# Attention and two experts in one kernel: a transposition moved by one step, a subtraction doubled, a store put ahead of a load

## The chip, the cores and the metric

One core of a Trainium2 chip runs the whole kernel. The metric is device microseconds of one execution. Engines are TensorE (PE, with PEld for its weight loads), VectorE (DVE), ScalarE (ACT), GpSimd (POOL) and SyncE (SP), which here only issues DMAs.

## What is computed

A recurrent attention over 768 time steps, for 4 x 8 heads of dimension 40, and behind it two dense experts over the 3072 tokens:

```python
for t in range(S):
    y[:, :, t] = einsum('bhd,bhde->bhe', rt, state)
    Sa = einsum('bhde,bhe->bhd', state, at)
    state = state * wt - einsum('bhd,bhe->bhde', Sa, bt) + einsum('bhd,bhe->bhde', vt, kt)
x = y as (3072, 320)
x = ((x @ w1) * (x @ w2)) @ w3 @ w_out          # 320 -> 1024 -> 1024 -> 320
out = relu(x @ w_in) ** 2 @ w_out2              # 320 -> 2048 -> 320
```

## The kernel before

**Attention** runs in 24 windows of 64 time steps; a window covers two of the four batches, 16 heads as 8 pairs. In a window the recurrence becomes triangular systems. VectorE scales and masks the operands (`scale_a`, `scale_bk`, `mask_ak`), `fill_lanes` spreads the 32x32 diagonal blocks over lanes, GpSimd inverts them there step by step (`invert`, 62 small instructions), and `turn_inverse(n)` on VectorE transposes the inverse of window n back into `invT`. TensorE multiplies by it in `make_u0(n)` and `make_u1(n)`. On TensorE `make_u0(n)` waits for `turn_inverse(n)` and also for `mask_ak(n+1)`.

**The experts** run in 6 tiles of 512 tokens. The first expert folds `w3 @ w_out` into one matrix, so that it has 8 hidden blocks (`a0` to `a7`, `b0` to `b7`) and its fold; the second has 16 hidden blocks (`c0` to `c15`) and its projection. Every value is split in a high and a low part (`_hi`, `_lo`) rounded to the fp32r format, and a product is summed from the parts. For a hidden block ScalarE takes a copy (`take`, into `left`), VectorE combines (`combine`), ScalarE rounds (`h_hi`), VectorE subtracts (`rest_hidden`, `h_lo`), and TensorE uses it two blocks later. `into_hidden` sums eight terms, the last with `x_lo` of the third block. The model dimension is 320, 2 x 128 + 64. Of the third block `x2T_hi` holds its 64 rows twice, in partitions 0 to 63 and 64 to 127; of the weights the lower half of these partitions holds the high part and the upper half the low part. `x2T_lo` holds the 64 low rows in partitions 0 to 63 and zeros above them.

**The order of work** is written out by hand. Each engine has a generator `experts()`, which yields 56 times in a tile, and a loop over windows 4 to 23 that draws 14 steps of it in each window with `next(beside)`. The first LEAD = 4 steps are empty. Windows 0 to 3 (the opening) stand before the loop, with the folding of `w3 @ w_out`. So the middle of a tile, where the first expert's result is turned into `x2T_hi` and `x2T_lo`, falls at the end of windows 5, 9, 13, 17 and 21, directly ahead of the next window's `scale_a`; the sixth tile's middle comes behind the windows.

**Weights** are rounded and split in the first tile, and written to DRAM for later tiles. A list `splits` gives each split a slot. SP issues all DMAs in its own order; `load_staged` brings raw weights into one of four `stage` buffers, four splits ahead (LOOK); ScalarE (`round_split`) and VectorE (`rest_of_split`) split them into `w_ring` or `v_ring`; `store_split` writes the result to `gate_rows`, `win_rows` or `wout_rows`. `pass_split(x)` on SP does both: the next load into the stage that x used, and the store of x. A load for a `w` split is four DMAs, for a `v` split one.

Lines that the text names: L1486 the transposition of `turn_inverse`; L1452 `scale_a` (`azk`); L1459 `scale_bk` (`bkT`); L1467 and L1471 `mask_ak`; L1556 and L1558 `combine`; L1250 and L1548 `h_hi` and `h_lo`; L1564 `rest_x`; L1590 the low part of the third block; L1239 `round_split` of a `v` split; L1535 and L1540 to L1542 `rest_of_split`; L866 `into_hidden`; L768 `make_u0` and `make_u1`; L811 `turn_uv`; L388 and L394 to L397 `load_staged`; L410 to L419 `store_split`; L429 `load_w`.

Of the kernel before, what the change touches and what calls it, by code (L numbers as in the profile page):

```python
# [5 lines left out]
F32 = mybir.dt.float32  # L6
F32R = mybir.dt.float32r
ALU = mybir.AluOpType
# [69 lines left out]
def attention_with_experts(nc, xT_dram, inputs, w1, w2, w3, w_out, w_in, w_out2, out):  # L78


    P, C, X, DP = 128, inputs.C, inputs.PAIRS, 64
# [7 lines left out]
    TOK = 512  # L89
    SUB, TILES = TOK // P, T // TOK  # L90
    REM = M - 2 * P
    DX = M + REM
    FT, FT2 = F // P, F2 // P
# [7 lines left out]
    OPENING = 4  # L101
# [12 lines left out]
    with ExitStack() as ctx:  # L114
# [3 lines left out]
        def sem(name):  # L118
            return ctx.enter_context(nc.semaphore(name))
# [84 lines left out]
        w_loaded = [sem(f"w_loaded{x}") for x in range(SLOTS)]  # L204
        v_loaded = [sem(f"v_loaded{x}") for x in range(SLOTS)]
        x_loaded, x_rounded, x_split = sem("x_loaded"), sem("x_rounded"), sem("x_split")
        third_rounded, third_split, third_cleared = sem("third_rounded"), sem("third_split"), sem("third_cleared")
        taken, combined, hi_made, lo_made, h_used, out_stored = (
            sem("taken"), sem("combined"), sem("hi_made"), sem("lo_made"), sem("h_used"), sem("out_stored"))

# [136 lines left out]
        def _(sp):  # L347
# [104 lines left out]
            W_LOADS, V_LOADS = TILES * (FT + FT2 // 2), TILES * (FT + FT2)  # L452

            def pass_split(x):
                _, kind, at = splits[x]
                if x + LOOK < len(splits):
                    sp.wait_ge(v_split if kind else w_split, at - FT + 1 if kind else at + 1)
                    load_staged(FT + x + LOOK)
                store_split(x)

            def split_first():
                for t, _ in enumerate(experts()):
# [223 lines left out]
        def _(pe):  # L686
# [273 lines left out]
            def experts():  # L960
                for _ in range(LEAD):
                    yield
                pe.wait_ge(y_scaled, OPENING)
                pe.wait_ge(st_copied, OPENING)
                for i in range(TILES):
                    def wait_x2(n):
                        if n in (0, 2):
                            wait_first_reader(pe, f"x{n // 2}", i)
                        elif n in (4, 5):
                            wait_drained(pe, f"x{n - 4}", i)  # L970
                        elif n == 6:
                            pe.wait_ge(third_rounded, 2 * (i + 1))
                        elif n == 7:
                            pe.wait_ge(third_split, i + 1)
                            pe.wait_ge(third_cleared, 1)

                    def wait_x(n):
                        if n in (0, 2):
                            pe.wait_ge(x_rounded, 3 * i + n // 2 + 1)
                        elif n in (4, 5):  # L980
                            pe.wait_ge(x_split, 3 * i + n - 3)
                        elif n == 6:
                            pe.wait_ge(x_rounded, 3 * (i + 1))
                        elif n == 7:
                            pe.wait_ge(x_split, 3 * (i + 1))

                    for f in range(FT + LAG):
                        if f < FT:
                            at = (FT + FT2 // 2) * i + f
                            wait_w(at)  # L990
                            for n, use in enumerate((f"a{f}", f"b{f}")):
                                (wait_left, wait_right)[n](f, i)
                                into_hidden(use, w_ring[at % SLOTS], 5 * P * n, xT_hi, xT_lo,
                                            *((wait_x,) if use == "a0" else ()))
                                yield
                        if f >= LAG:
                            fold(f - LAG, i)
                            yield
                    for f in range(FT2 + LAG):
                        if f < FT2:  # L1000
                            at = (FT + FT2 // 2) * i + FT + f // 2
                            wait_w(at)
                            wait_hidden(f, i)
                            into_hidden(f"c{f}", w_ring[at % SLOTS], 5 * P * (f % 2), x2T_hi, x2T_lo,
                                        *((wait_x2,) if f == 0 else ()))
                            yield
                        if f >= LAG:
                            project(f - LAG, i)
                            yield
# [152 lines left out]
        def _(act):  # L1162
# [158 lines left out]
                last = nc.scalar.copy(unit_rows[rows], ident[rows, rows].rearrange("i (x r) -> i x r", r=4).unsqueeze(  # L1321
                    3).broadcast_to([BLK, X, 4, X]))
            last.then_inc(unit_placed, 1)

            act.wait_ge(padded, 6)
            nc.scalar.copy(x2T_lo[REM:P, 2, :], zeros[REM:P].broadcast_to([REM, TOK])).then_inc(third_cleared, 1)
            copy_r(0)
            copy_w3(0)
            copy_blocks(0)
# [96 lines left out]
        def _(dve):  # L1426
# [140 lines left out]
            def experts():  # L1567
                for _ in range(LEAD):
                    yield
                for i in range(TILES):  # L1570
                    for f in range(FT + LAG):
                        if f < FT:
                            if 0 < f <= LAG:
                                rest_hidden(f - 1, i)
                            yield
                            combine(f, i)
                            yield
                        if f >= LAG:
                            if f < FT:
                                rest_hidden(f, i)  # L1580
                            if f == FT + LAG - 1:
                                wait_first_reader(dve, "x2", i)
                                drain(nc.vector.tensor_tensor(third[:], bank("x2")[0:REM], third[:], ALU.add), "x2", 1)
                                for m in range(2):
                                    wait_first_reader(dve, f"x{m}", i)
                                    drain(nc.vector.tensor_tensor(x2T_lo[:, m, :], bank(f"x{m}"),  # L1586
                                                                  x2T_hi[:, m, :].bitcast(F32), ALU.subtract),
                                          f"x{m}", 1)
                                dve.wait_ge(third_rounded, 2 * i + 1)
                                nc.vector.tensor_tensor(x2T_lo[0:REM, 2, :], third[:], x2T_hi[0:REM, 2, :].bitcast(F32),  # L1590
                                                        ALU.subtract).then_inc(third_split, 1)
                            yield
                    for f in range(FT2 + LAG):
                        if f < FT2:
                            if 0 < f <= LAG:
                                rest_hidden(FT + f - 1, i)
                            combine(FT + f, i)
                            yield
                        if f >= LAG:
                            if f < FT2:  # L1600
                                rest_hidden(FT + f, i)
                            if f == FT2 and i + 1 < TILES:
                                rest_x(i + 1)
                            if f == FT2 + LAG - 1:
                                wait(dve, out_stored, 16 * i)
                                for s in (1, 3):
                                    wait_filled(dve, f"o{s}", i)
                                    drain(nc.vector.tensor_copy(out_rows[:, s, :], bank(f"o{s}")[:, 0:M]), f"o{s}")
                            yield
# [84 lines left out]
            scale_a(5)  # L1694
            rest_of_fold(7)
            scale_bk(5)
            turn_inverse(OPENING)
            rest_x(0)
            for n in range(OPENING, WINDOWS):
                one, two = window_steps(n)  # L1700
                if OPENING < n and one:
                    scale_a(n + 1)
                next(beside)
                next(beside)
                if OPENING < n and one:
                    scale_bk(n + 1)
                next(beside)
                if one:
                    mask_ak(n + 1)
                    fill_lanes(n + 1)  # L1710
                next(beside)
                next(beside)
                next(beside)
                next(beside)
                add_x1(n)
                if two:
                    scan(n + 2)
                next(beside)
                if two:
                    invert_decay(n + 2, 0)  # L1720
                next(beside)
                if two:
                    invert_decay(n + 2, 1)
                next(beside)
                if two:
                    new_state(n)
                next(beside)
                mask_read(n)
                next(beside)
                scale_y(n)  # L1730
                next(beside)
                if one:
                    turn_inverse(n + 1)
                next(beside)
            for _ in beside:
                pass
# [31 lines left out]
```

## Time and profile before

| | before |
|---|---|
| median of 3 runs | 1060.74 us (1056.57 to 1061.88) |
| profiled execution | 1060.74 us, span 1059.0 us |
| TensorE busy | 1023.2 us, 97% |
| VectorE busy | 634.7 us, 60% |
| ScalarE busy | 419.7 us, 40% |
| GpSimd busy | 486.1 us, 46% |
| TensorE's granted clock, mean | 0.99 of full |

The profile is of one execution. A timeline row gives the start and the duration in us, the engine, the line, the operation with its output and inputs, and, in brackets, how long the engine had been idle before and what ended that. Where a row says x2 or x3, that many instructions are merged into it. A stretch's row gives its length, the busy time (and instructions) of PE, PEld, DVE, ACT and POOL, the granted clock, the busy share of the DMA engines and the GB/s that they moved.

### The profile page before, as it was taken

How to read it: one execution, taken by the hardware profiler on the slowest of the kernel's cores; microseconds unless marked ns; L12 is line 12 of the kernel's file. 1: busy time of each engine (PE TensorE's matmuls, PEld its weight loads, DVE VectorE, ACT ScalarE, POOL GpSimd, SP SyncE). 2: the span in 40 equal slices, each digit the busy share in tenths (PEclk: the TensorE clock that was granted, in tenths of full speed). 3: DMA queues.
4: the chain of work that ended last, by engine and by line, in shares of the span. 5: the costliest groups of instructions: out<-in, count | busy, mean ns of one | idle time of the engine just before them, and what ended most of it. 6: DMA issues, size and time to landing. Idle time of an engine off the chain costs nothing.

```text
span 1059.0 us, 27606 instructions
## 1 busy us (share of the span) xinstructions
PE 1023.2 (97%) x11008; PEld 880.8 (83%) x11008; DVE 634.7 (60%) x1005; ACT 419.7 (40%) x796; POOL 486.1 (46%) x1573
## 2 busy tenths in 40 slices
PE   5998989999999999999999999999999999999998
PEld 5786768779898888898888898888988888897797
DVE  6876366777875656666567566467567555442333
ACT  3453434454543343443344343334434234332332
POOL 4777755527447346346346355355365364200000
PEclk8997999999999999999999999999999999999999
DMA  9953556756886764757665757756648744555552
GB/s 177 188 127 65 155 132 170 197 165 203 226 234 178 170 150 126 180 145 180 151 157 131 176 140 202 150 134 155 160 125 217 154 117 132 154 169 184 166 170 75
DMA packets 267390, 169.05 MB, mean 160 GB/s; under 512 B 199680, under 2 KB 229376, under 8 KB 267264
## 3 DMA queue, kind: packets, MB, share of 16 engines
q1 hardware_dynamic: 267264, 167.29, 62.7%
q8 instruction: 88, 1.44, 0.6%
q14 instruction: 38, 0.31, 0.1%
HBM read 141.03 MB, written 26.21 MB: 158 GB/s over the span
## 4 chain that ended last, share of the span: by engine, by line
PE 79%; DVE 4%; ACT 2%; issue 1%; ACTq 0%; DVEq 0%
PE aside L866 31%; PE moe_bank L953 16%; PE moe_bank L938 8%; PE both L830 3%; PE both L730 3%; PE both L768 3%; PE both L840 2%; PE both L844 2%; PE both L760 2%; PE both L811 2%; PE both L743 1%; PE both L819 1%; PE both L793 1%; PE both L853 1%; PE both L716 1%
## 5 line engine op out<-in xcount | busy, mean ns | idle before, releaser
L671 POOL TENSOR_TENSOR inv_tmp<-blk,inv 128x60 f32<-128x60 f32 (+24 forms) x744 | 209.5, 282 | 358.4 <-DVE blk L1480 301.4
L675 POOL TENSOR_TENSOR inv<-inv,inv_tmp 128x60 f32<-128x60 f32 (+24 forms) x744 | 237.4, 319 | 58.3
L953 PE MATMUL moe_bank<-v_ring,h_hi 128*128 128x320 f32 x768 | 175.3, 315 | 0.0
L866 PE MATMUL aside<-x2T_hi,w_ring 128*128 128x512 f32 x480 | 148.0, 405 | 4.4 <-DVE h_lo L1548 4.3
L866 PE MATMUL aside<-xT_hi,w_ring 128*128 128x512 f32 x480 | 148.2, 406 | 2.2 <-DVE h_lo L1548 1.5
L1558 DVE SCALAR_TENSOR_TENSOR aside<-aside,left 128x512 f32<-128x512 f32 x96 | 66.9, 697 | 122.0 <-ACT left L1258 122.0
L953 PEld LDWEIGHTS moe_bank<-v_ring,h_hi 128*128 128x128 f32 x768 | 128.0, 188 | 3.9
L1548 DVE TENSOR_TENSOR h_lo<-aside,h_hi 128x512 fp32r<-128x512 f32 x144 | 97.4, 677 | 49.7 <-ACT h_hi L1250 49.0
L1250 ACT CAST h_hi<-aside 128x512 fp32r<-128x512 f32 x144 | 84.7, 588 | 94.9 <-DVE aside L1558 49.6
L953 PE MATMUL moe_bank<-v_ring,h_lo 128*128 128x320 f32 x384 | 118.6, 309 | 0.0
L1258 ACT ACTIVATE left<-aside 128x512 f32<-128x512 f32 x96 | 57.4, 598 | 117.3 <-PE aside L866 117.3
L866 PEld LDWEIGHTS aside<-x2T_hi,w_ring 128*128 128x128 f32 x480 | 84.1, 188 | 21.3 <-issue 6.3
L866 PEld LDWEIGHTS aside<-xT_hi,w_ring 128*128 128x128 f32 x480 | 84.7, 188 | 19.2 <-DVE h_lo L1548 2.6
L866 PE MATMUL aside<-xT_lo,w_ring 128*128 128x512 f32 x288 | 97.1, 391 | 0.0
L866 PE MATMUL aside<-x2T_lo,w_ring 128*128 128x512 f32 x288 | 96.9, 391 | 0.0
L1438 DVE RECIPROCAL undecay<-decay 104x256 f32<-104x256 f32 x48 | 83.2, 1739 | 0.2
L938 PE MATMUL moe_bank<-h_hi,v_ring 128*128 128x512 f32 x240 | 81.4, 404 | 0.0
L953 PEld LDWEIGHTS moe_bank<-v_ring,h_lo 128*128 128x128 f32 x384 | 72.1, 188 | 0.0
L1556 DVE TENSOR_TENSOR aside<-left,aside 128x512 f32<-128x512 f32 x48 | 33.0, 687 | 63.1 <-PE aside L866 63.1
L866 PEld LDWEIGHTS aside<-xT_lo,w_ring 128*128 128x128 f32 x288 | 54.1, 188 | 12.8 <-DVE xT_lo L1564 0.6
L866 PEld LDWEIGHTS aside<-x2T_lo,w_ring 128*128 128x128 f32 x288 | 54.1, 188 | 12.3 <-DVE x2T_lo L1586 0.2
L1197 ACT COPY uv<-both 32x320 f32<-32x320 f32 x88 | 36.8, 418 | 68.9 <-PE both L768 63.4
(151 smaller groups left out, 1604.2 us busy)
## 6 DMA issues: line engine op xcount, KB each, us to landing
w_ring<-gate_rows SPq DMA_DIRECT2D x40, 640.0 KB, 4.6
w_ring<-win_rows SPq DMA_DIRECT2D x40, 640.0 KB, 4.1
v_ring<-wout_rows SPq DMA_DIRECT2D x80, 320.0 KB, 3.1
v_ring<-fold_rows SPq DMA_DIRECT2D x48, 320.0 KB, 4.2
gate_rows<-w_ring SPq DMA_DIRECT2D x8, 640.0 KB, 6.4
win_rows<-w_ring SPq DMA_DIRECT2D x8, 640.0 KB, 4.4
wout_rows<-v_ring SPq DMA_DIRECT2D x16, 320.0 KB, 5.9
stage<-in_moe_w SPq DMA_DIRECT2D x8, 512.0 KB
```

The costliest lines, as they stand in the source:

```text
L671: nc.gpsimd.tensor_tensor(tmp, x[:, j, 0:j].unsqueeze(2).broadcast_to([P, j, X - lo]), mine[:, j:j + 1, lo:X].broadcast_to([P, j, X - lo]) ...
L675: nc.gpsimd.tensor_tensor(mine[:, 0:j, lo:X], mine[:, 0:j, lo:X], tmp, ALU.add).then_inc(solve, 1)
L866: last = nc.tensor.matmul(bank(use), w, x, start=n == 0, stop=n == len(terms) - 1)
L938: last = nc.tensor.matmul(bank(f"x{m}"), weights[:, lo:lo + P], h[at % RING][:], start=f == 0 and n == 0, stop=f == FT - 1 and n == len(te ...
L953: last = nc.tensor.matmul(bank(f"o{s}")[:, 0:M], h[at % RING][:, s * P:(s + 1) * P], weights[:, rest * M:(rest + 1) * M], start=f == 0 and ...
L1197: last = nc.scalar.copy(uv[n % 2][rows, :, q, 0:D], by_head(its_first(n), rows))
L1250: nc.scalar.copy(h_hi[at % RING][:], hidden_at(x)).then_inc(hi_made, 1)
L1258: nc.scalar.activation(left[x % 2][:], hidden_at(x), ACT.Relu).then_inc(taken, 1)
L1438: nc.vector.reciprocal(undecay[0:E, xs], decay[n % 4][0:E, xs, 1:C + 1]).then_inc(undecayed, 1)
L1548: nc.vector.tensor_tensor(h_lo[at % RING][:], hidden_at(x), h_hi[at % RING][:].bitcast(F32), ALU.subtract).then_inc(lo_made, 1)
L1556: nc.vector.tensor_tensor(into, left[x % 2][:], into, ALU.mult).then_inc(combined, 1)
L1558: nc.vector.scalar_tensor_tensor(out=into, in0=into, scalar=0.0, in1=left[x % 2][:], op0=ALU.max, op1=ALU.mult).then_inc(combined, 1)
```

## The change

Four edits.

- `x2T_lo` of the third block is no longer zero in partitions 64 to 127. VectorE writes the 64 low rows a second time, there; ScalarE's copy of zeros at the start, with its semaphore `third_cleared`, is gone, and `third_split` counts two for each tile. TensorE's last term then adds the product of both low parts as well.
- In `pass_split` the store of split x is issued before the staged load of x + 4.
- `turn_inverse(n)` in the window loop moves from the end of window n-1 (between its last two steps) to window n, behind `scale_a(n+1)` and one step.
- `turn_inverse(4)`, which stood ahead of `rest_x(0)`, is now the first of these, in window 4, behind `rest_x(0)`.

```diff
--- before.py
+++ after.py
@@ -204,7 +204,7 @@
         w_loaded = [sem(f"w_loaded{x}") for x in range(SLOTS)]
         v_loaded = [sem(f"v_loaded{x}") for x in range(SLOTS)]
         x_loaded, x_rounded, x_split = sem("x_loaded"), sem("x_rounded"), sem("x_split")
-        third_rounded, third_split, third_cleared = sem("third_rounded"), sem("third_split"), sem("third_cleared")
+        third_rounded, third_split = sem("third_rounded"), sem("third_split")
         taken, combined, hi_made, lo_made, h_used, out_stored = (
             sem("taken"), sem("combined"), sem("hi_made"), sem("lo_made"), sem("h_used"), sem("out_stored"))
 
@@ -452,11 +452,9 @@
             W_LOADS, V_LOADS = TILES * (FT + FT2 // 2), TILES * (FT + FT2)
 
             def pass_split(x):
-                _, kind, at = splits[x]
+                store_split(x)
                 if x + LOOK < len(splits):
-                    sp.wait_ge(v_split if kind else w_split, at - FT + 1 if kind else at + 1)
                     load_staged(FT + x + LOOK)
-                store_split(x)
 
             def split_first():
                 for t, _ in enumerate(experts()):
@@ -971,8 +969,7 @@
                         elif n == 6:
                             pe.wait_ge(third_rounded, 2 * (i + 1))
                         elif n == 7:
-                            pe.wait_ge(third_split, i + 1)
-                            pe.wait_ge(third_cleared, 1)
+                            pe.wait_ge(third_split, 2 * (i + 1))
 
                     def wait_x(n):
                         if n in (0, 2):
@@ -1321,9 +1318,6 @@
                 last = nc.scalar.copy(unit_rows[rows], ident[rows, rows].rearrange("i (x r) -> i x r", r=4).unsqueeze(
                     3).broadcast_to([BLK, X, 4, X]))
             last.then_inc(unit_placed, 1)
-
-            act.wait_ge(padded, 6)
-            nc.scalar.copy(x2T_lo[REM:P, 2, :], zeros[REM:P].broadcast_to([REM, TOK])).then_inc(third_cleared, 1)
             copy_r(0)
             copy_w3(0)
             copy_blocks(0)
@@ -1587,8 +1581,10 @@
                                                                   x2T_hi[:, m, :].bitcast(F32), ALU.subtract),
                                           f"x{m}", 1)
                                 dve.wait_ge(third_rounded, 2 * i + 1)
-                                nc.vector.tensor_tensor(x2T_lo[0:REM, 2, :], third[:], x2T_hi[0:REM, 2, :].bitcast(F32),
-                                                        ALU.subtract).then_inc(third_split, 1)
+                                for q in range(2):
+                                    nc.vector.tensor_tensor(x2T_lo[REM * q:REM * (q + 1), 2, :], third[:],
+                                                            x2T_hi[0:REM, 2, :].bitcast(F32), ALU.subtract).then_inc(
+                                                                third_split, 1)
                             yield
                     for f in range(FT2 + LAG):
                         if f < FT2:
@@ -1694,13 +1690,13 @@
             scale_a(5)
             rest_of_fold(7)
             scale_bk(5)
-            turn_inverse(OPENING)
             rest_x(0)
             for n in range(OPENING, WINDOWS):
                 one, two = window_steps(n)
                 if OPENING < n and one:
                     scale_a(n + 1)
                 next(beside)
+                turn_inverse(n)
                 next(beside)
                 if OPENING < n and one:
                     scale_bk(n + 1)
@@ -1729,8 +1725,6 @@
                 next(beside)
                 scale_y(n)
                 next(beside)
-                if one:
-                    turn_inverse(n + 1)
                 next(beside)
             for _ in beside:
                 pass
```

## Rows read from the trace of the kernel before

**Rows 1.** The page, part 4: shares of the span in the chain that ended last.
```profile
PE 79%; DVE 4%; ACT 2%; issue 1%; ACTq 0%; DVEq 0%
```

**Rows 2.** The transpositions by tile (ns min/median/max), and the waits: us, times, longest.
```profile
L1486 DVE STREAM_TRANSPOSE invT<-inv x24: 656/688/715, 46.2 to 910.1; 128x256 f32<-128x256 f32 x24
...
DVE invT L1486 <- POOL inv L675: 6.1, 2, 4.7
...
PE both L730 <- DVE bkT L1459: 3.9, 4, 1.3
```

**Rows 3.** VectorE's timeline at two window edges: start, duration, instruction, [idle before].
```profile
426.20 0.70 DVE L1558 SCALAR_TENSOR_TENSOR aside<-aside,left 128x512 f32<-128x512 f32 x1 [2.58 <-ACT left L1258]
426.81 0.68 DVE L1486 STREAM_TRANSPOSE invT<-inv 128x256 f32<-128x256 f32 x1
427.56 0.69 DVE L1548 TENSOR_TENSOR h_lo<-aside,h_hi 128x512 fp32r<-128x512 f32 x1
...
350.61 0.70 DVE L1556 TENSOR_TENSOR aside<-left,aside 128x512 f32<-128x512 f32 x1 [2.32 <-PE aside L866]
```

**Rows 4.** Timelines of VectorE and TensorE in the middle of the second tile.
```profile
387.82 0.68 DVE L1590 TENSOR_TENSOR x2T_lo<-third,x2T_hi 64x512 fp32r<-64x512 f32 x1
388.43 1.40 DVE L1452 SCALAR_TENSOR_TENSOR azk<-both,decay 64x512 f32<-64x512 f32 x2
390.24 0.70 DVE L1558 SCALAR_TENSOR_TENSOR aside<-aside,left 128x512 f32<-128x512 f32 x1 [0.41 <-ACT left L1258]
391.60 0.69 DVE L1548 TENSOR_TENSOR h_lo<-aside,h_hi 128x512 fp32r<-128x512 f32 x1 [0.66 <-ACT h_hi L1250]
...
388.85 0.40 PE L866 MATMUL aside<-x2T_lo,w_ring 128*128 128x512 f32 x1
...
392.43 1.17 PE L866 MATMUL aside<-x2T_hi,w_ring 128*128 128x512 f32 x4 [0.49 <-DVE h_lo L1548]
```

**Rows 5.** Timelines of VectorE and TensorE where the opening ends.
```profile
145.60 1.90 DVE L1564 TENSOR_TENSOR xT_lo<-x_raw,xT_hi 128x512 fp32r<-128x512 f32 x3 [2.15 <-ACT xT_hi L1265]
147.53 0.86 DVE L1467 COPY diag<-both 32x256 f32<-32x256 f32 x2
...
150.07 0.76 PE L768 MATMUL both<-x_row,invT 32*32 32x40 f32 x32 [2.01 <-DVE azk L1471]
```

**Rows 6.** VectorE's timeline around a weight split in the first tile.
```profile
156.84 0.69 DVE L1540 TENSOR_TENSOR w_ring<-stage,w_ring 128x512 fp32r<-128x512 f32 x1 [1.31 <-ACT w_ring L1242]
157.55 0.45 DVE L1542 TENSOR_TENSOR w_ring<-stage,w_ring 64x256 fp32r<-64x256 f32 x1
158.03 0.99 DVE L1493 TENSOR_TENSOR x_row<-both,x_row 32x320 f32<-32x320 f32 x2
```

**Rows 7.** Timelines in the middle of the first tile and of the last.
```profile
222.96 0.49 DVE L1535 TENSOR_TENSOR v_ring<-stage,v_ring 128x320 fp32r<-128x320 f32 x1 [0.36 <-ACT v_ring L1239]
...
996.50 0.67 DVE L1590 TENSOR_TENSOR x2T_lo<-third,x2T_hi 64x512 fp32r<-64x512 f32 x1
...
997.40 0.39 PE L866 MATMUL aside<-x2T_lo,w_ring 128*128 128x512 f32 x1
```

**Rows 8.** Timelines of SP's queue, ScalarE and TensorE, a wait, and the stretch 286 to 289.
```profile
282.57 0.43 SPq L388 DMA_DIRECT2D stage<-in_moe_w_out  x1
283.05 0.43 SPq L419 DMA_DIRECT2D win_rows<-w_ring  x1
...
287.57 0.46 ACT L1239 CAST v_ring<-stage 128x320 fp32r<-128x320 f32 x1 [2.30 <-DMA stage<-in_moe_w_out]
288.05 0.85 ACT L1197 COPY uv<-both 32x320 f32<-32x320 f32 x2
...
289.00 1.05 PE L811 MATMUL both<-ident,uv 128*104 128x128 f32 x8 [0.51 <-issue]
...
ACT v_ring L1239 <- DMA stage<-in_moe_w_out: 2.3, 1, 2.3
...
286.00:289.00 3.00, 2.49 (x36) 1.81 (x29) 2.96 (x8) 1.37 (x4) 2.53 (x7) 1.00 1.01 373
```

## The prediction

> **What bounds the kernel now.** I read the page first, then the waits, then the timelines of the engines around each place that the diff touches. The page's chain that ended last is TensorE's for 79% of the span, VectorE's for 4% and ScalarE's for 2% [rows 1]. So a VectorE or ScalarE instruction matters only where TensorE stands still behind it; the question for each edit is whether it lands in a gap of VectorE or ahead of something TensorE waits for. In the timeline of TensorE, idle times over 0.2 us are few after 145 us, and they recur. One comes at every middle of a token tile, when the second expert's `c2` waits for `h_lo` of `c0` (0.49 us in four tiles, [rows 4]); the others are in the opening and in the first tile, where the weights are also split.
>
> The profiled execution took 1060.74 us, 1059.0 of them span; it is also the median of the three runs (1056.57 to 1061.88), so I add to 1060.74.
>
> **The change part by part.**
>
> *The transposition `turn_inverse`, moved in the window loop.* It takes about 0.69 us, 24 times [rows 2]. Before, it stood ahead of the last beside-step of window n-1; now it stands behind `scale_a(n+1)` and one beside-step of window n. Old place: in the windows that end inside the second expert it sits between `combine` and `rest_hidden`, where VectorE has to wait for ScalarE's rounding. In [rows 3], `combine` starts at 426.20, the transposition at 426.81, `h_lo` at 427.56: 1.36 us from combine to `h_lo`. At 390.24 there is no transposition and `h_lo` starts at 391.60, again 1.36 us [rows 4]. So it costs nothing where it is. New place: for window starts that fall in the second expert the first beside-step of the window is again a `combine`, and the next begins with `rest_hidden`, so the same gap takes it. For the window starts inside the first expert the step behind it is a `combine` that VectorE waits 2.32 us for [rows 3]. Cost nothing, gain nothing; without that cover it would be 0.6 us for each of 19 windows, 11 us. Its reader, `make_u0(n)`, waits for `mask_ak(n+1)` anyway, and that stands behind the transposition on VectorE in both orders, so no new wait comes in. VectorE's waits for GpSimd's inversion are 6.1 us in total, two of them [rows 2]; the longer one (4.7 us) is in the opening before the loop and stays, the other comes at the end of a first-expert stage, ahead of the wait for ScalarE's copy of `third`, so removing it frees nobody.
>
> *The same transposition in the opening.* `turn_inverse(4)` stood ahead of `rest_x(0)`. There VectorE idled 2.15 us for ScalarE's `xT_hi` [rows 5], so it was free. Now it comes behind `rest_x(0)` and in front of `mask_ak(5)`, with only empty steps between (LEAD is 4). `mask_ak(5)` starts at 147.53 directly behind the last `xT_lo`, and TensorE's `make_u0(4)` at 150.07 has been idle 2.01 us for exactly that result (`azk`, L1471) [rows 5]. One transposition, started back to back, is 0.6 us: **+0.6 us**, all exposed.
>
> *A second subtraction for the last 64 rows of `x2T_lo`, six times.* It replaces one ScalarE copy of zeros at the start, when TensorE still waits for its first DMA: gain nothing. The existing subtraction takes 0.68 us (387.82 in [rows 4]), and the instruction after it starts 0.61 us later, since the two overlap. The new one writes partitions 64 to 127. [Rows 6] shows a pair of that kind: an op of 0.69 us, the one on partitions 64 to 127 starting 0.71 us later, and the next 0.48 us after that for a duration of 0.45: no overlap into it, none out of it. So I count 0.80 us until the next VectorE instruction, not 0.61. (The Trainium skill, VectorE: DVE Perf Modes, section "Two Vector instructions with no wait between them", gives a model in which an instruction whose output begins in another quadrant of partitions than the last one's is held until the earlier ones have finished; [rows 6] agrees. If it did not hold here, the four middle tiles would cost 0.6 us each in place of 0.8.)
> What waits behind it, in the four middle tiles: TensorE's eighth term of `c0`, which started at 388.85 with the old subtraction finished at 388.50, must wait until about 389.25 (0.4 us); and `scale_a`, which moves from 388.43 to 389.23. ScalarE's second `copy_r` piece needs the first half of `scale_a`, and `take(c0)` is queued behind it on ScalarE, then `combine` (390.24), `h_hi`, `h_lo` (391.60), then TensorE's `c2` at 392.43, which already waits 0.49 us [rows 4]. That whole chain moves by 0.8, so **4 x 0.8 = +3.2 us**. In the first tile a weight split lies between, for which VectorE idled 0.36 us [rows 7]: 0.70 less 0.36, **+0.35 us**. In the last tile there is no `scale_a`: the subtraction at 996.50 ends at 997.17, the second would end at about 997.86, and TensorE's term started at 997.40 [rows 7]: **+0.5 us**.
>
> *The order in `pass_split`: store before next load.* The same waits, and the same issues on SP's queue: a store moves ahead of one or four loads. Every store comes 0.5 to 2 us earlier; in the trace nobody waits for one of these stores. Every staged load is issued one store later and its bytes line up behind the store's. ScalarE rounds staged weights 32 times and idles for a load before one of them alone [rows 8]: that load was issued at 282.57 and rounded at 287.57 after 2.30 us of idling for it. The copies of `uv` for which `turn_uv` waits are queued behind that rounding (288.05), and TensorE starts `turn_uv` at 289.00 after 0.51 us idle. So this delay is exposed already. With the new order the 640 KB store of `win_rows` (now issued at 283.05) goes in front of the load: 655,360 B at the 373 GB/s that the row of this stretch shows are 1.8 us, with the DMA engines as good as full (1.01) [rows 8]. I take **+1.8 us**; bounds are 0 (bytes of both interleave and the load still lands in time) and 4 (this load and the next one both late by as much). (The Trainium skill, DMA: Bandwidth & Descriptors, section "Queues, rings and completion order", says that each DMA engine takes the descriptors of a ring in order, which would put the load fully behind the store; the wait at 287.57 fits that but doesn't prove it.)
>
> **Sum:** 0.6 + 3.2 + 0.35 + 0.5 + 1.8 = 6.45 us. 1060.74 + 6.45 = **1067.2 us**, 0.6% slower. A measurement of this kernel can tell about 0.5% (5.3 us) from no change, so this lies just beyond the line.
>
> **Rivals.**
> 1. *The load isn't held up by the store.* For it: the two directions differ, and the load before took no more than 5 us in all. Against: saturated engines. Then 4.65 us remain: 1065.4, within 0.5%.
> 2. *The added subtraction is half covered.* TensorE waits only for its own eighth term (0.4 us at 388.85) and ScalarE's chain catches up, because the second `copy_r` piece has slack. Against it: `azk` starts without a gap at 388.43. Then 4 x 0.4 in place of 4 x 0.8: 1065.6; with rival 1 together 1063.8. Within 0.5%.
> 3. *More staged loads come late.* In the first tile the waits of SP's queue leave some loads little time, as this one shows, and only the latest is seen in the waits of before; if three of them become late by a store each (1.8 us), the time is 1067.2 + 3.6 = 1070.8.
> 4. *Faster, by taking the transposition out of the end of the window.* If it delays `scale_a` and with it `bkT` and `cross`, TensorE's waits for `bkT` go, 3.9 us in four places [rows 2]; with all 6.1 us of VectorE's waits for GpSimd given back as well that is 10.0 us, less the 4.65 above: 1055.4. It decides if the transposition that waited for GpSimd inside the loop holds up `scale_a` and the chain to `c2`. Against it: VectorE idles for ScalarE or TensorE in the gaps where the transpositions stand [rows 3].
>
> **How the numbers follow.** Forecast (load late, subtraction exposed) 0.44, of which 0.38 over the line of 5.3 us; rival 1 0.19; rival 2, alone or with 1, 0.18; rival 3 0.11; rival 4 0.08. Slower by over 0.5%: 0.38 + 0.11 = 0.49. Within 0.5%: 0.06 + 0.19 + 0.18 = 0.43. Faster by over 0.5%: 0.08, rival 4, whose full price just reaches the line. The range leaves out rival 4 and the top of rival 3: 1061.5 (rivals 1 and 2 together, less half the spread of the runs before) to 1071.0. The forecast's own range is 1065.5 to 1069.
>
> **What would show it.** In the profile after: TensorE's wait before `c2` in the middle tiles grows from 0.49 to about 0.9 us, plus about 0.4 us before the eighth term of `c0`, both behind VectorE; `azk` starts about 1.4 us behind the first of the two subtractions instead of 0.6. The wait before `make_u0(4)` goes from 2.01 to 2.6 us. `h_lo` still starts 1.36 us behind `combine` where the transposition now lies between. ScalarE's wait for the staged output weights goes from 2.3 to about 4 us and TensorE's wait before that `turn_uv` from 0.5 to 2.3. The prediction is wrong if the middle-tile wait stays near 0.5, if the staged wait stays or goes, or if a transposition shows up in front of something TensorE waits for.

## The result and the profile after

The changed kernel takes 1068.25 us (median of 6 runs, 1066.61 to 1071.19) against 1060.6 us before (6 runs, 1056.57 to 1061.88): ratio 1.0081, 95% interval 1.0057 to 1.0105. In a second series it gave 1069.42 us against 1061.49, ratio 1.0088 (1.0068 to 1.0109). It is slower, by 8.6 to 9.3 us by the ratios (7.7 and 7.9 by the medians) where 6.45 were forecast. The profiled execution after took 1071.43 us, 1069.6 of them span, so it is above all six of its own runs, and differences read from it are at their upper end.

The page of the changed kernel, its engines and the chain that ended last:

```profile
PE 1026.7 (96%) x11008; PEld 882.2 (82%) x11008; DVE 639.1 (60%) x1011; ACT 418.8 (39%) x795; POOL 483.7 (45%) x1573
...
PE 78%; DVE 5%; issue 2%; ACT 1%; ACTq 0%; DVEq 0%
```

TensorE has the same instructions and stands still for longer; VectorE has six more, ScalarE one less. In the chain TensorE and ScalarE have one point less each, VectorE and "issue" (time in which an engine waits for nothing that the profile shows) one more ([rows 1] for before).

The largest single loss in this profile does not come from VectorE. Timelines of SP's queue, of ScalarE and of TensorE in the changed kernel, where [rows 8] are those of before, and the two stretches that follow:

```profile
282.69 0.58 SPq L429 DMA_DIRECT2D w_ring<-gate_rows  x1
283.32 0.43 SPq L419 DMA_DIRECT2D win_rows<-w_ring  x1
283.79 0.47 SPq L388 DMA_DIRECT2D stage<-in_moe_w_out  x1
...
291.79 0.46 ACT L1236 CAST v_ring<-stage 128x320 fp32r<-128x320 f32 x1 [6.51 <-DMA stage<-in_moe_w_out]
292.27 0.85 ACT L1194 COPY uv<-both 32x320 f32<-32x320 f32 x2
...
293.22 1.92 PE L809 MATMUL both<-ident,uv 128*104 128x128 f32 x8 [4.72 <-issue]
...
292.00:299.00 7.00, 5.78 (x46) 5.43 (x48) 5.48 (x6) 3.54 (x7) 5.67 (x18) 0.51 0.85 309
299.00:1060.00 761.00, 754.62 (x7801) 653.88 (x7796) 434.11 (x669) 288.37 (x543) 298.52 (x991) 1.00 0.60 156
```

The store is issued ahead of the load now. The load, issued at 283.79, is rounded by ScalarE 8.0 us later, 5.0 before; ScalarE idles 6.51 us for it instead of 2.30, and TensorE stands still for 4.72 us instead of 0.51. Then comes something that was not in the forecast: TensorE's granted clock, at full speed before (2.4 GHz), is 0.51 in the stretch from 292 to 299, so about 1.2 GHz, and full again from 299 on. The eight transpositions at 293.22 take 1.92 us; those of before at 289.00 took 1.05 [rows 8].

The middle of the second tile, timelines of VectorE and TensorE in the changed kernel ([rows 4] for before):

```profile
394.53 1.40 DVE L1585 TENSOR_TENSOR x2T_lo<-third,x2T_hi 64x512 fp32r<-64x512 f32 x2
395.97 1.41 DVE L1446 SCALAR_TENSOR_TENSOR azk<-both,decay 64x512 f32<-64x512 f32 x2
397.79 0.70 DVE L1552 SCALAR_TENSOR_TENSOR aside<-aside,left 128x512 f32<-128x512 f32 x1 [0.41 <-ACT left L1255]
398.52 0.67 DVE L1480 STREAM_TRANSPOSE invT<-inv 128x256 f32<-128x256 f32 x1
399.15 0.69 DVE L1542 TENSOR_TENSOR h_lo<-aside,h_hi 128x512 fp32r<-128x512 f32 x1
...
395.99 0.50 PE L864 MATMUL aside<-x2T_lo,w_ring 128*128 128x512 f32 x1 [0.26 <-DVE x2T_lo L1585]
399.99 1.17 PE L864 MATMUL aside<-x2T_hi,w_ring 128*128 128x512 f32 x4 [0.79 <-DVE h_lo L1542]
```

From the first subtraction to `azk` it is 1.44 us, 0.61 before: 0.83 more for the second one. From the first subtraction to TensorE's `c2` it is 5.46 us, 4.61 before: 0.85 us for this tile, and the three tiles after it repeat it (0.26 and 0.76 or 0.77 us of waiting). TensorE's idle time grows by less, 0.26 before the eighth term and 0.30 before `c2`; the rest is that matmuls which overlapped no longer do: the eighth term starts 0.65 us behind the one ahead of it and the next 0.34 us behind the eighth, where both distances were 0.23 us before. The transposition lies between `combine` (397.79) and `h_lo` (399.15), which start 1.36 us apart as before.

Where the opening ends, in the changed kernel ([rows 5] for before):

```profile
146.54 0.69 DVE L1480 STREAM_TRANSPOSE invT<-inv 128x256 f32<-128x256 f32 x1
147.27 0.86 DVE L1461 COPY diag<-both 32x256 f32<-32x256 f32 x2
...
149.81 0.76 PE L766 MATMUL both<-x_row,invT 32*32 32x40 f32 x32 [2.63 <-DVE azk L1465]
```

The transposition pushes `mask_ak(5)` back, and TensorE waits 2.63 us for `azk`, 2.01 before. TensorE still starts `make_u0(4)` no later than before (149.81 against 150.07): this start lies between 147.7 and 151.3 us in the fourteen profiles, so in this profile the 0.6 us show only in the wait.

### The profile page after: what moved, and what is told of

Same layout as the page of the kernel before. It is cut to its first block, busy times and chain, and to the rows that moved or that the text cites. A ratio compares the mean times of both kernels' runs of the same rounds, so it can differ in the third digit from the quotient of the medians.

```text
span 1069.6 us, 27605 instructions
## 1 busy us (share of the span) xinstructions
PE 1026.7 (96%) x11008; PEld 882.2 (82%) x11008; DVE 639.1 (60%) x1011; ACT 418.8 (39%) x795; POOL 483.7 (45%) x1573
## 3 DMA queue, kind: packets, MB, share of 16 engines
q8 instruction: 88, 1.44, 0.6%
## 4 chain that ended last, share of the span: by engine, by line
PE 78%; DVE 5%; issue 2%; ACT 1%; ACTq 0%; DVEq 0%
PE aside L864 31%; PE moe_bank L951 16%; PE moe_bank L936 8%; PE both L828 3%; PE both L728 3%; PE both L766 3%; PE both L838 2%; PE both L842 2%; PE both L758 2%; PE both L809 2%; PE both L741 1%; PE both L817 1%; PE both L791 1%; PE both L851 1%; PE both L714 1%
## 5 line engine op out<-in xcount | busy, mean ns | idle before, releaser
L673 POOL TENSOR_TENSOR inv<-inv,inv_tmp 128x60 f32<-128x60 f32 (+24 forms) x744 | 234.9, 316 | 58.3
```

The source lines that it names most:

```text
L673: nc.gpsimd.tensor_tensor(mine[:, 0:j, lo:X], mine[:, 0:j, lo:X], tmp, ALU.add).then_inc(solve, 1)
```

## The experiments

Each kernel was run beside the kernel before on the same chip. The last columns come from the profiled execution: ScalarE's longest idle time for a staged load, TensorE's before `turn_uv` behind it, and TensorE's granted clock from 149 to 156 us, where the opening ends. ("e1" is `e1_store_first`, and so on.)

| kernel | ratio to before | 95% interval | ScalarE's wait, us | TensorE's wait, us | clock, opening |
|---|---|---|---|---|---|
| before | 1 | | 2.3 | 0.5 | 1.00 |
| changed | 1.0081 | 1.0057 to 1.0105 | 6.5 | 4.7 | 1.00 |
| e5, changed, second series | 1.0088 | 1.0068 to 1.0109 | 4.4 | 2.65 | 1.00 |
| e1, order in `pass_split` alone | 1.0021 | 1.0006 to 1.0036 | 4.8 | 3.1 | 0.52 |
| e6, the order of one split alone | 1.0034 | 1.0016 to 1.0053 | 5.0 | 3.3 | 1.00 |
| e2, second subtraction alone | 1.0037 | 1.0021 to 1.0053 | 1.5 | none | 0.76 |
| e3, transpositions alone | 1.0000 | 0.9987 to 1.0013 | 1.9 | none | 0.83 |
| e7, e1 and e2 together | 1.0062 | 1.0038 to 1.0087 | 4.3 | 2.5 | 0.76 |
| e4, changed, but for one split's order | 1.0039 | 1.0027 to 1.0051 | 1.6 | none | 0.58 |
| e10, changed, with one load early | 1.0041 | 1.0024 to 1.0058 | 0.5, another load | none | 0.54 |
| e9, before, with that load early | 0.9999 | 0.9985 to 1.0013 | none | none | 1.00 |
| e8, second subtraction on other rows | one run, 1067.26 us | | 2.9 | 1.1 | 0.76 |
| e11, first transposition alone | one run, 1063.50 us | | 2.3 | 0.5 | 0.52 |
| e12, transpositions in the loop alone | one run, 1061.97 us | | 3.4 | 1.6 | 1.00 |

One run is too few for a ratio; of e8, e11 and e12 only the rows of the profile are used.

**The store first, in all splits (e1_store_first).**

```diff
-                if x + LOOK < len(splits):
-                    sp.wait_ge(...)
-                    load_staged(FT + x + LOOK)
                 store_split(x)
+                if x + LOOK < len(splits):
+                    load_staged(FT + x + LOOK)
```

The wait that goes (its arguments are left out here) stands in `store_split` too, for the same split.

> Only the order in pass_split is changed. Theory (the store holds up the one staged load that was late already): TensorE's wait before turn_uv grows from 0.5 to 3 to 5 us, behind it the granted clock falls to half for some us, and the time is 4 to 7 us above before (1.004 to 1.007). Nothing else in the trace moves by over 1 us. Rival (stores earlier are worth something, and the loss came from VectorE's edits): the wait stays under 1 us and the time is that of before or under it.

Measured: 1.0021 (2.2 us), half of what the theory expected at least, and its interval (up to 1.0036) leaves that out. The waits are there, on ScalarE and TensorE in its profile:

```profile
ACT v_ring L1237 <- DMA stage<-in_moe_w_out: 4.8, 1, 4.8
...
294.02 1.06 PE L809 MATMUL both<-ident,uv 128*104 128x128 f32 x8 [3.06 <-issue]
```

In this execution the clock did not fall behind the wait: from the wait for `bkT` at 274.14 to `c2` at 397.45 it is 123.31 us, 120.77 in the trace of before, 2.54 more, as much as the wait itself grew (3.06 less 0.51). So the fall is no sure companion of the wait. (It did fall in the opening of this execution; the last section has the rows.) The rival, that stores earlier are worth something, fell.

**The second subtraction alone (e2_low_twice).** The diff is that of the change in `rest`, `wait_x2` and at ScalarE's start.

> Only the second subtraction into x2T_lo, and no zeros at the start. Theory: 0.35 + 4 x 0.8 + 0.5 = 4.1 us above before (1.004); azk starts 1.43 us behind the first of the two subtractions instead of 0.61; TensorE waits 0.26 us before the eighth term of c0 and 0.77 us before c2 in the four middle tiles. Rival (half covered): about 2 us.

Measured: 1.0037, 3.9 us. TensorE's waits in its profile, in the second tile and in the last:

```profile
390.59 0.50 PE L866 MATMUL aside<-x2T_lo,w_ring 128*128 128x512 f32 x1 [0.24 <-DVE x2T_lo L1587]
394.58 1.16 PE L866 MATMUL aside<-x2T_hi,w_ring 128*128 128x512 f32 x4 [0.78 <-DVE h_lo L1544]
...
1002.57 0.50 PE L866 MATMUL aside<-x2T_lo,w_ring 128*128 128x512 f32 x1 [0.39 <-DVE x2T_lo L1587]
```

The theory holds in size and place. In the profile the added time is 0.37 us in the first tile (between the waits for `bkT` at 189 and 274 us it is 84.92 us, 84.55 before), 0.82 to 0.84 in each middle tile and 0.61 in the last, 4.3 us in all. Half covered (2 us, 1.0019) lies just below the interval, and the 0.82 us rule it out.

**The transpositions alone (e3_turn_moved).** `turn_inverse(4)` goes behind `rest_x(0)`, and `turn_inverse(n)` behind the first step of window n.

> Only turn_inverse is moved, in the loop and out of the opening. Theory: 0.6 us above before, all of it before make_u0(4), where TensorE's wait goes from 2.0 to 2.6 us; every h_lo behind a transposition still starts 1.36 us behind its combine. Rival (a transposition lies ahead of what TensorE waits for): 0.6 us for each window, up to 11 us. Rival (faster): TensorE's waits for bkT shrink by up to 2.6 us.

Measured: 1.0000. The wait before `make_u0(4)` is there:

```profile
147.73 1.10 PE L768 MATMUL both<-x_row,invT 32*32 32x40 f32 x32 [2.62 <-DVE azk L1471]
```

but 0.6 us are within what the interval (1.3 parts in a thousand, 1.4 us) can't see. Both rivals at their full price, 11 us slower and 2.6 us faster, are excluded.

**The changed kernel, with one split in the old order (e4_after_but_one).**

```diff
 def pass_split(x):
+    if x == 23:      # load_staged(FT + 27) ahead of the store, as before
+        ...
```

> The changed kernel, but for one of the 32 splits (the 24th, whose staged load was issued at 282.57 in the trace of before) the load goes ahead of the store as before. Theory (that one pair carries the whole DMA cost): the wait before turn_uv is back at about 0.5 us, no fall of the clock, and the time is 4.7 us above before (1.0045) instead of 8.5. Rival (the order matters in many places): the wait moves to another staged load and the time stays near that of the changed kernel.

Measured: 1.0039. One reordered pair accounts for the difference to the changed kernel, 0.0042 or 4.5 us (give or take 2.8, from both intervals). ScalarE still waits for that load, as little as in other profiles with the old order, and TensorE doesn't wait before `turn_uv`:

```profile
290.62 0.46 ACT L1243 CAST v_ring<-stage 128x320 fp32r<-128x320 f32 x1 [1.56 <-DMA stage<-in_moe_w_out]
```

No other load has become late.

**The changed kernel again (e5_after_again), one split alone (e6_one_split), and two of the three parts (e7_low_and_store).** e6 is the kernel before with `if x == 23:` store first, and e7 is e1 and e2 in one.

> The changed kernel once more, beside its parts. The three parts alone gave 1.0021, 1.0037 and 1.0000, together 1.0058, while the changed kernel gave 1.0081 (1.0057 to 1.0105). Theory (they add up): 1.005 to 1.007. Rival (the parts act on each other, above all through the wait for the staged load): 1.008 or more again.

> The kernel before, with store ahead of load for the 24th split alone. Theory (this pair carries the whole cost of the reordering): the same as with all splits reordered, 1.002, with TensorE's wait before turn_uv at 2.5 to 5 us and ScalarE's wait for the staged load at 4 to 6.5. Rival (the load is late through the sum of the reordered pairs ahead of it): the wait stays near 0.5 us and the time that of before.

> The second subtraction and the order in pass_split, without the moved transpositions. Theory (parts add): 1.006. If the parts act on each other: 1.008 as in the changed kernel, with the transpositions innocent; if 1.006 here and 1.008 there, the transpositions matter together with the rest.

Measured: 1.0088, 1.0034, 1.0062. The one reordered pair costs as much as all of them (1.0034 against 1.0021, intervals that overlap). The theory for e5, that the parts simply add up to at most 1.007, was too low; its rival got the number. With e6 for the reordering, the parts alone give 1.0034 + 0.0037 + 0 = 1.0071, inside both intervals of the changed kernel; with e1 it is 1.0058, at the lower edge of one and outside the other. Whether the parts act on each other by some 2 us or the runs scatter by that is not settled. The granted clock is a candidate, since in a profile it can cost that much. The stretch behind the wait, in the profiles of e5 and e6 (length, busy times, granted clock, DMA share, GB/s):

```profile
292.00:296.00 4.00, 4.00 (x28) 3.68 (x27) 4.00 (x5) 1.88 (x4) 3.22 (x11) 0.57 1.04 369
```

```profile
292.00:296.00 4.00, 4.00 (x20) 3.83 (x17) 4.00 (x5) 2.12 (x4) 3.22 (x11) 0.57 1.03 388
```

The granted clock fell in both, and in the changed kernel's first profile; it did not in those of e1 and e7. What it costs comes from the stretch between the wait for `bkT` at about 272 us and `c2` of the next tile. In the changed kernel it is 128.31 us, 7.54 more than before; 4.21 of it is the wait, 0.85 the subtraction, and 2.48 are left, with a fall that lasts from 292 to 299. In e6 it is 125.07 us: 4.30 more, 2.75 of wait, 1.55 left. In e5 1.5 is left as well (125.28), and in e7 nothing (123.57: 2.80 more, 1.99 of wait and 0.83 of subtraction).

Over all runs the clock explains less. Each run, profiled or not, gives its mean granted clock. Among the 35 runs of the kernel before beside e1 to e4, the four with a mean of 0.993 or more took 1056.35 to 1059.26 us, the four with 0.988 1062.84 to 1064.74: some 0.8 us for each thousandth. So the clock is behind much of the scatter of one kernel's runs. Between kernels it hardly differs: 0.9899 on average before (0.9899 and 0.9902 in the later series), 0.9897 in the changed kernel, 0.9890 in e5, 0.9896 in e1, 0.9900 in e6, 0.9901 in e7, and 0.9892 in e9, which has no such wait at all. At 0.8 us a thousandth that is at most 0.7 us of e5's time over before, and 0.9 us of the 2.3 us between e5 and e7.

**The second subtraction on other partitions (e8_low_same_rows).** The output of the second subtraction is 64 rows of `xT_lo` in partitions 0 to 63, which nobody reads at that time; the zeros stay.

```diff
+ for q in range(2):
+     nc.vector.tensor_tensor((x2T_lo[0:REM, 2, :], xT_lo[0:REM, 2, :])[q], third[:], ...)
```

> As the kernel with the second subtraction, but it writes to partitions 0 to 63 of a tile that is free at that moment, and the zeros stay. Theory (an output on other partitions keeps the instruction and the next from overlapping their neighbours): azk starts 1.22 us behind the first subtraction, not 1.43, and TensorE waits 0.2 us less before c2, 0.57. Rival (the price is the instruction's own): 1.43 and 0.77 as with the other partitions.

VectorE's timeline in its profile, and TensorE's `c2`:

```profile
391.43 0.68 DVE L1591 TENSOR_TENSOR x2T_lo<-third,x2T_hi 64x512 fp32r<-64x512 f32 x1
392.04 0.68 DVE L1591 TENSOR_TENSOR xT_lo<-third,x2T_hi 64x512 fp32r<-64x512 f32 x1
392.64 1.40 DVE L1452 SCALAR_TENSOR_TENSOR azk<-both,decay 64x512 f32<-64x512 f32 x2
...
396.64 1.16 PE L866 MATMUL aside<-x2T_hi,w_ring 128*128 128x512 f32 x4 [0.64 <-DVE h_lo L1548]
```

`azk` starts 1.21 us behind the first subtraction, not 1.44, and TensorE no longer waits before the eighth term; before `c2` it waits 0.64 us, 0.07 more than expected. From the first subtraction to `c2` it is 5.21 us against 5.46. So in this tile 0.25 us are the price of the partitions and 0.60 of the instruction. (The Trainium skill, VectorE: DVE Perf Modes, section "Two Vector instructions with no wait between them", has this hold; 1.44 against 1.21 us agrees with it.)

**The late load issued early, in both kernels (e9_early_load, e10_after_early_load).** A repair:

```diff
                 if n % 4 == 3:
                     load_x(n // 4, 0)
+                if n == 7:
+                    sp.wait_ge(w_split, splits[23][2] + 1)
+                    load_staged(FT + 23 + LOOK)
```

and `pass_split(23)` leaves the load out.

> The kernel before, with the staged load of the 28th split (the one that ScalarE waited for) issued ahead of window 9's four bk loads, two to four us earlier. Theory (only this load is short of time): ScalarE's wait for a staged load is gone and so is TensorE's wait before turn_uv; 0 to 1 us faster, 0.999 to 1.000. Rival (another load or the bk loads become late): a new wait at turn_bk or at another rounding, 1 us or more slower.

> The changed kernel with the same early load. Theory (the reordering costs through this load alone): the time falls from 1.008 to what the second subtraction and the opening cost, 1.0045, as in the run that left out one split; no fall of the granted clock behind 285 us. Rival (other pairs cost as well): 1.006 or more.

Measured: 0.9999 and 1.0041. In e9 the load is issued at 279.66 and ScalarE rounds without a wait for it:

```profile
279.66 0.35 SPq L388 DMA_DIRECT2D stage<-in_moe_w_out  x1
...
285.20 0.46 ACT L1242 CAST v_ring<-stage 128x320 fp32r<-128x320 f32 x1
...
288.36 1.03 PE L814 MATMUL both<-ident,uv 128*104 128x128 f32 x8
```

In the changed kernel this alone gives back 0.0047, 5 us of e5's ratio (give or take 2.8), and what is left, 4.3 us, is near what the second subtraction (4.3) and the opening (0.6) cost by the profiles. ScalarE waits 0.47 us for a later load in e10, and TensorE for none. Behind 285 us the clock stays full in both. On the kernel before it can't be told from nothing, and no version found here beats the kernel before.

**The two moves of the transposition, one run each (e11_turn_opening, e12_turn_loop).**

> Only turn_inverse(4) is moved behind rest_x(0); the loop is as before. Theory: TensorE's wait before make_u0(4) goes from 2.0 to 2.6 us and nothing else moves. Rival (VectorE catches up in the windows that follow): the 0.6 us is given back before 190 us.

> Only the transpositions in the loop are moved; turn_inverse(4) stays ahead of rest_x(0). Theory: the wait before make_u0(4) stays 2.0 us; h_lo starts 1.36 us behind its combine with a transposition between; the waits before c2 stay at 0.45 to 0.5 us and the one for bkT at 187 us shrinks by 0.1. Rival: waits for h_lo or bkT grow by up to 0.6 us.

TensorE where the opening ends, in e11 and then in e12:

```profile
150.21 1.28 PE L768 MATMUL both<-x_row,invT 32*32 32x40 f32 x32 [2.63 <-DVE azk L1471]
```

```profile
150.25 0.76 PE L768 MATMUL both<-x_row,invT 32*32 32x40 f32 x32 [2.02 <-DVE azk L1471]
```

The 0.6 us come from the opening alone. In e12 the wait for `bkT` at 187 us is 0.43 us (0.56 in e11), and `c2` in the second tile waits 0.51 us: nothing is paid in the loop. In e11 nothing before 190 us gives the time back. But the theory that nothing else moves did not hold in this one execution: from `make_u0(4)` to the wait for `bkT` it is 39.73 us, 37.04 before and 36.92 in e12, with TensorE's clock at half behind the wait:

```profile
149.00:156.00 7.00, 5.79 (x46) 4.85 (x47) 4.47 (x6) 2.51 (x5) 3.32 (x11) 0.52 0.83 203
```

Nothing ties this to the moved transposition: e1, without the move, shows the same, and e5 and the changed kernel's own profile, with it, don't.

## Why the prediction held, and its one mis-sized term

The sign, the places and the range were right (1068.25 us within 1061.5 to 1071.0; 1067.2 forecast). Term by term:

| term | forecast, us | measured |
|---|---|---|
| transpositions in the loop | 0 | 0: e12's waits, e3's ratio |
| `turn_inverse(4)` behind `rest_x(0)` | 0.6 | 0.6 in the wait; not visible in a ratio |
| second subtraction, all tiles | 3.2 + 0.35 + 0.5 = 4.05 | 3.9 by e2's ratio, 4.3 in its profile |
| store ahead of load | 1.8, bounds 0 and 4 | by ratios 2.2 (e1), 2.7 (e7 less e2), 3.6 (e6), 4.5 (changed less e4), 5.0 (e5 less e10); 2.7 of waiting by the profiles, without the clock |

The mis-sized step is the last, "I take +1.8 us". The mechanism was the one told, and the place too: one load, of the 28 that are issued behind a store now. Each of the five figures from ratios is uncertain by 1.6 to 3.1 us, and only e5 less e10 leaves 1.8 out by itself; but all five lie above it, and so do the profiles. In seven profiles that have this load ahead of the store (before, e2, e3, e4, e8, e11, e12) ScalarE waits 1.5 to 3.4 us for it, 2.3 on average, and TensorE 0 to 1.6, 0.5 on average. In the five with the store first ScalarE waits 4.3 to 6.5 us, 5.0 on average, and TensorE 2.5 to 4.7, 3.2 on average. So TensorE's wait grows by 2.7 us and not by 1.8. The 2.3 us of [rows 8] were a typical value; the size of the delay was wrong. I priced it as 640 KB at the rate of the stretch. From issue to rounding the load takes 7.4 us on average in the five profiles and 5.1 in the seven, 2.3 more, and its issue comes about 0.5 us later, since the store's own issue stands ahead of it on SP's queue (283.32 to 283.79), for which the sum had nothing. Why 640 KB cost 2.3 us and not 1.8 stays open: the rates were much the same (343 and 410 GB/s from 286 to 289 and from 289 to 292 us in the changed kernel, 373 and 371 before).

The forecast also had no term for the granted clock. In three of the five profiles with the long wait TensorE ran at half clock for some microseconds behind it, worth 1.5 to 2.5 us; in the changed kernel's profile wait and fall together are 4.21 + 2.48 = 6.7 us, over the upper bound of 4. But the mean clocks of all runs leave at most 0.7 us for it. With the 2.7 us of waiting that makes up to 3.4 us, in the middle of the five ratios. The parts so read come to at most 0.6 + 4.3 + 3.4 = 8.3 us, inside the intervals of both series of the changed kernel, whose own values are 8.6 and 9.3.

That 1068.25 us lies so near the 1067.2 of the forecast owes a little to luck: the term for the store was too small by 1 to 3 us, and the median of the first series shows less of that than its ratio. The range's lower end was worked out wrongly, too: 1063.8 less half the spread of the runs before (2.65) is 1061.15 and not 1061.5.

Of the signs named beforehand, the opening's wait (2.6), the 1.4 us to `azk`, the 1.36 us to `h_lo` and the growth of a middle tile (0.85 against 0.8) came as told. The waits themselves were smaller than told (0.26 and 0.79 against 0.4 and 0.9), as overlap was lost as well. (The 0.80 us "until the next VectorE instruction" is the time added by the second subtraction, as the sum uses it; 0.83 were measured.)

Rival 1 (the load isn't held up) fell with e1, e6 and the waits. Rival 2 (half covered) fell with e2. Rival 3 (more loads late) did not happen: only one is late for TensorE, but by more (e4, e10). Rival 4 fell with e3 and e12: `bkT`'s waits stay at 3.7 us (3.9 before, [rows 2]).

## What to carry to other kernels

In an in-order queue, look for the one transfer that is late already, and ask what a reorder puts in front of it; the other 27 reordered loads of this kernel cost nothing that a ratio shows (e4 and e10 against e2). An instruction moved or added on an engine that is 60% busy costs nothing in a gap that ends with another engine's result, and its full length if it stands between two results that the bound engine waits for in turn. One profile's wait for a DMA is a sample: the same kernel waited 6.5 us in one profile and 4.4 in another. Look at several executions, and at the mean clock of all runs, before pricing a change by it.

## What was not expected of the hardware

A wait of 2.65 to 4.7 us by TensorE in the middle of a dense stretch was followed by half its clock in three profiles (0.51 from 292 to 299 us, 0.57 from 292 to 296) and by none in two (waits of 2.5 and 3.1 us), so in one execution a wait of that size may cost half as much again. (The Trainium skill, TensorE: Matmul & The Clock Gate, Part 1, says that the clock is set by how busy TensorE has been recently; all three falls come behind a wait, which agrees. That waits of the same size go without a fall in other executions is what these profiles add.) The same chance sits in the opening. Behind the 2.0 us wait at 150 us the profile of before shows full clock, and e1's, whose wait is as long (2.02 us), a half:

```profile
148.00:155.00 7.00, 4.99 (x56) 4.26 (x56) 5.52 (x8) 3.70 (x7) 2.64 (x8) 1.00 0.82 217
```

```profile
149.00:156.00 7.00, 6.52 (x49) 5.58 (x50) 3.78 (x5) 2.19 (x5) 3.89 (x13) 0.52 0.86 216
```

The first row is of before, the second of e1. Eight of the fourteen profiles show a fall there, with waits of 2.0 or 2.6 us alike, and it has a price: from the start of `make_u0(4)` to that of the matmuls at 186 to 191 us that wait for `bkT` (L730) it is 36.9 to 37.1 us in the six profiles without a fall and 38.5 to 40.1 in the eight with one, 1.5 to 3.1 us more. That is a large part of the 5 us over which one kernel's runs scatter. Of the five profiles with the long wait, the three that fell behind it are the three that had kept full clock in the opening, which would explain why the mean clock of those kernels is hardly lower. Five profiles are too few to show it.
